# Block-local attention and two MoE layers on one core: scores moved to tiles 0, 2, 4 of every block, heads on 64 rows, two buffers for queries with keys and for values, low halves of w_in on VectorE

## The reference

```
q_c = q[:, :, c_start:c_end]                      # 4 x 8 heads, 768 tokens, head size 64
k_full = concat([mem_k, k[l_start:r_end]])        # 64 keys a chunk; v_full likewise
scores = scale * q_c @ k_full.T; scores -= max(scores)
a = exp(scores); a = a / (sum(a) + 1e-9); x_c = a @ v_full
h = x @ w_in                                      # 3072 x 512 @ 512 x 2048
g = h * cos(h);  y = g @ w_out                    # 2048 x 512
h2 = max(max(y @ w1, y @ w2), y @ w3)             # 512 x 768 each
out = h2 @ w_out2                                 # 768 x 512
```

## Time and profile before

| | |
|---|---|
| median of 3 runs | 1000.99 us (997.13 to 1005.64) |
| profiled execution | 1001.07 us, span 999.3 us |
| granted TensorE clock, mean | 0.991 |
| busy: TensorE, VectorE, ScalarE, GpSimd | 96%, 68%, 52%, 21% |
| first tile of block 0 starts | 30.71 us |
| last evacuation of the first stage | 393.6 us |

### The profile page before, as it was taken

One profiled execution on the slowest core, in us unless ns is written; L12 is line 12 of the kernel. 1 busy time (PEld: TensorE's weight loads), 2 busy tenths in 40 slices (PEclk: granted clock), 3 DMA queues, 4 the chain that ended last, 5 costly groups with the idle time before them and its releaser, 6 DMA issues.

```text
span 999.3 us, 18401 instructions
## 1 busy us (share of the span) xinstructions
PE 955.4 (96%) x7564; PEld 927.5 (93%) x7564; DVE 675.2 (68%) x926; ACT 516.5 (52%) x689; POOL 213.3 (21%) x231
## 2 busy tenths in 40 slices
PE   5779999999999999999999999999999999999998
PEld 4678889898989899999999999999999999999998
DVE  4355666566665678998998989866646446677761
ACT  1576786767777789443343335443323224344441
POOL 3341111112111221200200000763000001684510
PEclk7999999999999999999999999999999999999999
DMA  9993656574754444343445433332020121334532
GB/s 206 218 241 101 173 149 191 146 201 128 203 151 146 142 134 168 126 156 109 159 144 183 146 114 122 127 137 74 32 95 32 65 95 53 117 116 139 179 116 85
DMA packets 65395, 135.41 MB, mean 136 GB/s; under 512 B 5920, under 2 KB 27424, under 8 KB 65312
## 3 DMA queue, kind: packets, MB, share of 16 engines
q1 hardware_dynamic: 54944, 98.58, 33.8%
q0 software_dynamic: 10368, 35.66, 10.9%
HBM read 87.03 MB, written 47.19 MB: 134 GB/s over the span
## 4 chain that ended last, share of the span: by engine, by line
PE 72%; ACT 10%; DVE 8%; DMA 5%; issue 3%; SPq 2%; POOL 1%; DVEq 0%; ACTq 0%
PE ps L606 23%; PE ps L608 22%; PE ps L607 22%; DMA early_qk<-qk_in 2%; PE ps L622 2%; ACT work L912 2%; DMA g_dram<-work 2%; DVE work L1189 2%; ACT work L914 1%; DVE units L1226 1%; PE ps L647 1%; ACT work L907 1%; ACT work L904 1%; PE ps L656 1%; DVE ssum L1156 1%
## 5 line engine op out<-in xcount | busy, mean ns | idle before, releaser
L606 PE MATMUL ps<-units 128*128 128x384 f32 (+1 forms) x1940 | 609.4, 314 | 6.7 <-ACT work L1087 3.0
L608 PE MATMUL ps<-units 128*128 128x384 f32 (+1 forms) x1940 | 602.3, 310 | 0.0
L607 PE MATMUL ps<-units 128*128 128x384 f32 (+1 forms) x1940 | 601.8, 310 | 0.0
L606 PEld LDWEIGHTS ps<-units 128*128 128x128 f32 x1940 | 368.5, 190 | 17.5 <-issue 5.6
L607 PEld LDWEIGHTS ps<-units 128*128 128x128 f32 x1940 | 368.7, 190 | 0.0
L608 PEld LDWEIGHTS ps<-units 128*128 128x128 f32 x1940 | 368.6, 190 | 0.0
L932 ACT CAST units<-work 128x1024 fp32r<-128x1024 f32 x96 | 85.7, 939 | 119.0 <-DVE work L1212 102.8
L1087 ACT COPY work<-ps 128x384 f32<-128x384 f32 (+1 forms) x144 | 63.5, 454 | 144.0 <-PE ps L608 143.8
L1184 DVE SCALAR_TENSOR_TENSOR work<-work 128x768 f32<-128x768 f32 x64 | 62.1, 970 | 73.4 <-ACT work L907 73.4
L1226 DVE TENSOR_TENSOR units<-work,units 128x1024 fp32r<-128x1024 f32 x96 | 102.6, 1110 | 10.9 <-ACT units L932 10.9
L494 POOL DMA_DIRECT2D g_dram<-work x64 | 46.7, 730 | 292.0 <-DVE work L1189 287.3
(11 more groups left out here) (96 smaller groups left out, 840.7 us busy)
## 6 DMA issues: line engine op xcount, KB each, us to landing
g_dram<-work POOLq DMA_DIRECT2D x64, 384.0 KB, 3.2
work<-g_dram SPq DMA_DIRECT2D x48, 512.0 KB, 3.8
work<-qk_in SPq DMA_DIRECT2D x36, 384.0 KB, 5.5
work<-v_in SPq DMA_DIRECT2D x40, 256.0 KB, 5.1
work<-w_in POOLq DMA_DIRECT2D x40, 256.0 KB, 3.6
h_dram<-work SPq DMA_DIRECT2D x24, 384.0 KB, 2.9
work<-h_dram SPq DMA_DIRECT2D x18, 512.0 KB, 3.9
work<-y_dram SPq DMA_DIRECT2D x8, 768.0 KB, 6.0
```

The source lines that it names most:

```text
L606: pe.matmul(o, wh, mh, start=start, stop=False, skip_group_check=onto)
L607: pe.matmul(o, wh, ml, start=False, stop=False, skip_group_check=onto)
L608: return pe.matmul(o, wl, mh, start=False, stop=stop, skip_group_check=onto)
```

## The change

- A score and a value matmul serve one head on its own 64 rows, 32 moving matmuls a token tile instead of 16, each with 64 moving columns instead of 128. The two heads write two banks (4 and 5; scores in their first, weighted values in their second halves). No zeros are needed, the rows of queries and keys are packed (384 numbers a pair of heads), and a token tile's load is one DMA.
- Every block computes the scores of the next block's token tiles at its tiles 0, 2 and 4, the exponentials ahead of the evacuation at tile 5, the rest of the attention at tiles 7 to 13.
- Token tiles from 9 on use two buffers for queries with keys and two for values. The order of the loads is new.
- The transposed probabilities have one bank (6) after the start, the transposed output bank 7.
- `low_wi` runs on VectorE, in the order `LOW_WI`; `high_wi` runs in the order `HIGH_WI`, w_in tile g at tile f of block 0. GpSimd stores only.
- Some steps of the weights of the next stage move by a few tiles.

```diff
+HIGH_WI = (0, 0, 0, 0, 0, 0, 0, 0, 1, 1, 2, 3, 3, 4, 4, 4)
+LOW_WI = (0, 0, 0, 0, 0, 0, 1, 1, 2, 3, 3, 4, 5, 6, 6, 8)
...
+        def by_head(n, half):
+            if n == 1:
+                banks, at = ps[:, 0:2, :], 0
+            elif n == 2:
+                banks, at = ps[:, 2:4, :], 0
+            else:
+                banks, at = ps[:, 4:6, :], 256 * half if n else 0
+            return banks[:, :, at:at + 256].rearrange("p r (a k) -> p a r k", a=PAIRS)
...
-                        mm = pe.matmul(scores(n)[chunk, a, :, :], q[:, a, KC + CH * c:KC + CH * c + CH],
-                                       two_parts(q, a, c, KC + SUB), start=True, stop=True)
+                        for r in range(2):
+                            mm = pe.matmul(scores(n)[chunk, a, r, :], queries_in(n, a, r, c), keys_in(n, a, r, c),
+                                           start=True, stop=True)
...
-                        mm = pe.matmul(weighted(n)[chunk, a, :, :], prob_t(n)[:, a, chunk],
-                                       values_in(n, a, c), start=True, stop=True)
+                        for r in range(2):
+                            mm = pe.matmul(weighted(n)[chunk, a, r, :], prob_t(n)[head_rows(r), a, chunk],
+                                           values_in(n, a, r, c), start=True, stop=True)
...
             def load_qk(n):
...
-                for r, columns in enumerate((slice(0, KC + SUB), slice(KC, 2 * KC + SUB))):
-                    rows = slice(P // 2 * r, P // 2 * (r + 1))
-                    sp.dma_start(qk_at(n)[rows, :, columns], qk_in[n, rows, :].rearrange("p (a x) -> p a x", a=PAIRS))\
-                      .then_inc(qk_sem(n)[0], 16)
+                sp.dma_start(qk_at(n), qk_in[n, :, :].rearrange("p (a x) -> p a x", a=PAIRS)).then_inc(qk_sem(n)[0], 16)
...
             load_qk(0)
             load_qk(1)
             load_v(0)
-            load_wi(0)
             load_qk(2)
             load_v(1)
             load_v(2)
-            for f in range(1, 6):
+            for f in range(4):
                 load_wi(f)
             for n in range(NSUB, 2 * NSUB):
                 load_qk(n)
-                load_wi(2 * n)
-                load_wi(2 * n + 1)
...
+                load_wi(2 * n - 2)
+                load_wi(2 * n - 1)
+            load_wi(10)
+            load_wi(11)
+            load_v(NSUB)
+            load_wi(12)
+            load_v(NSUB + 1)
+            load_wi(13)
+            load_v(NSUB + 2)
+            load_wi(14)
+            load_wi(15)
...
+            def attend(t, f):
+                n = NSUB * (t + 1)
+                if f in (0, 2, 4):
+                    scores_of(n + f // 2, n)
                 elif f == 7:
                     turn_probs(n)
                 elif f == 9:
-                    values(n)
+                    values(n, n + 3)
                     turn_probs(n + 1)
                 elif f == 10:
                     turn_out(n)
                     turn_probs(n + 2)
                 elif f == 11:
-                    values(n + 1)
-                    scores_of(n + NSUB)
+                    values(n + 1, n + 3)
                 elif f == 12:
                     turn_out(n + 1)
-                    scores_of(n + NSUB + 1)
+                    values(n + 2, n + 3)
                 elif f == 13:
-                    values(n + 2)
-                elif f == 14:
                     turn_out(n + 2)
-                    scores_of(n + NSUB + 2)
...
             for t in range(NBLK):
                 n = NSUB * (t + 1)
...
+                    if not last and f == 5:
                         exps(0, NSUB, n + NSUB)
                     if f % 2:
                         i = FPAIRS * t + f // 2
                         evacuate(i)
...
+                        if not last:
+                            if f == 7:
+                                copy_probs(n)
+                            elif f == 9:
+                                copy_probs(n + 1)
+                            elif f == 13:
+                                x_high(n + 2)
                         if i:
                             cosine(i - 1)
-                    if first:
+                    if t == 0:
+                        for g in range(4, NF):
+                            if HIGH_WI[g] == f:
+                                high_wi(g)
+                    if not last:
                         if f == 10:
                             x_high(n)
                             copy_probs(n + 2)
                         elif f == 12:
                             x_high(n + 1)
...
-                    if 1 <= t < 6 and f == 10:
+                    if 1 <= t < 6 and f == 8:
                         high_w1(t - 1)
```

More of the change, by code:

```diff
@@ L555, in _ @@
             pool.wait_ge(const_ready, 1)
[L556 to L565, removed]
+            for i in range(TILES):
                 store_g(i)
                 t, p = divmod(i, FPAIRS)
-                if 1 <= t < 5 and p == 6:
+                if t < 5 and p == (6 if t else 4):
                     load_w1(t)
@@ L978, in _ @@
             copy_probs(0)
-            high_wi(0)
             exps(2, 3, 3)
             copy_probs(1)
+            copy_probs(2)
+            high_wi(0)
+            high_wi(1)
             x_high(0)
-            copy_probs(2)
+            high_wi(2)
+            high_wi(3)
             x_high(1)
             x_high(2)
-            for f in range(1, 5):
-                high_wi(f)
             for t in range(NBLK):
                 n = NSUB * (t + 1)
-                first, last = t == 0, t == NBLK - 1
+                last = t == NBLK - 1
                 for f in range(NF):
-                    if first and f + 5 < NF:
-                        high_wi(f + 5)
-                    if first and f == 5:
+                    if not last and f == 5:
                         exps(0, NSUB, n + NSUB)
@@ L1268, in _ @@
             sums(0, 1, 1)
+            sums(1, 2, 2)
             shift(2)
-            sums(1, 2, 2)
             normalise(0)
@@ L1273, in _ @@
             normalise(1)
+            low_wi(0)
             x_low(0)
             normalise(2)
+            low_wi(1)
             x_low(1)
             x_low(2)
+            low_wi(2)
+            low_wi(3)
             for t in range(NBLK):
                 n = NSUB * (t + 1)
-                first, last = t == 0, t == NBLK - 1
+                last = t == NBLK - 1
                 for f in range(NF):
-                    if first:
-                        if f == 0:
-                            shift(n)
-                        elif f == 2:
-                            shift(n + 1)
-                        elif f == 4:
-                            shift(n + 2)
-                        elif f == 8:
-                            sums(0, NSUB, NSUB + 1)
+                    if not last:
+                        if f in (0, 2, 4):
+                            shift(n + f // 2)
+                        elif f == 5:
+                            sums(0, NSUB, NSUB + t + 1)
                         elif f == 9:
@@ L1294, in _ @@
                             normalise(n + 1)
-                            shift(n + NSUB)
-                        elif f == 13:
-                            normalise(n + 2)
-                    elif not last:
-                        if f == 2:
-                            sums(0, NSUB, NSUB + t + 1)
-                        elif f == 3:
-                            normalise(n)
-                        elif f == 7:
-                            normalise(n + 1)
-                        elif f == 11:
-                            normalise(n + 2)
                     if f % 2:
@@ L1309, in _ @@
                         turn(i)
+                        if f == 13 and not last:
+                            x_low(n + 2)
                         if i:
                             gated(i - 1)
-                    if first:
+                    if not last:
                         if f == 10:
```

233 lines of the change are left out of this document (76 added, 157 removed).

## The result

| | before | after |
|---|---|---|
| median | 999.76 us (997.13 to 1005.64, 4 runs) | 975.38 us (974.13 to 976.64, 4 runs) |
| ratio to before | | 0.9752, interval 0.9716 to 0.9788 |
| profiled execution | 1001.07 us, span 999.3 | 974.13 us, span 972.3 |

What follows compares the result with a forecast made beforehand. TensorE, busy 96%, was taken to set the pace after about 70 us, with full transfers before. Terms of -11, -5.4 and +1.4 gave -15 against 1001.07 us: 986 us, range 978 to 1018.

Steps and rivals of the forecast that it cites:

- Part 3: Start and block 0: 1.4 us more, bounds 4 us less to 6 more.
- the landing of w_in: Start: last part of w_in lands at 58 us again, bounds 55 and 61.
- What hung on that term: Block 0: ScalarE's conversions of w_in, last at 58.6 us, then exponentials and evacuation (62.9), so tile 8 starts at 63.
- the idle time before it: Block 0: TensorE idle for 14 us before tile 8.
- Rival D: Start: w_in's last pair lands at 62 to 65 us and holds ScalarE longer; time 1004 to 1008, chance 0.13.
- Part 1: Scores and values on 64 rows: slot of a group 0.7 us, down from 1.01, 36 times, 11 us less.
- rivals B and C: Score and value groups: B, row halves take turns, 997 us, chance 0.22; C, records set the pace, 1011 to 1029, 0.18.
- Part 2: New order in blocks 1 to 6: 2 us less, 1 less in each of 2 to 5, 0.6 more; 5.4 less in sum.
- the wait for VectorE: Blocks 1 to 6: the output's transposes no longer wait, as the normalisation comes at 14.4 us, before they want it at 14.5.
- the copy's wait: Blocks of the new order: the third probabilities' transposes wait for ScalarE's copy, a new wait of 1.5 us.
- the values' wait: Blocks of the new order: copy of the probabilities done at 10.95 us, wanted by the values at 10.9.

Runs made afterwards that it cites:

- halves: Kernel after, with each load of queries and keys or of values as two DMAs, on the lower and the upper 64 rows: 990.16 us, ratio 0.9912.
- evenodd: Kernel after, with each such load as two DMAs of 64 rows, one on the even and one on the odd rows: 976.54 us, ratio 0.9764.
- small: Kernel after, with queries and keys loaded over all 128 rows in pieces of 1.5 KB: 975.11 us, ratio 0.9755.
- before_two_queues: Kernel before, with DMAs of the upper 64 rows of token tiles 0 to 5 issued by ScalarE's queue: 1003.72 us, ratio 1.003.
- before_even_odd: Kernel before, with head 0 on even and head 1 on odd rows, zeros written ahead of the first loads: 996.78 us, ratio 0.9963.
- w1_at_10: Kernel after, with the high part of w_out back from tile 8 to tile 10 of blocks 1 to 5: 970.43 us, ratio 0.969.
- before_even_odd_low: before_even_odd with the low halves of w_in on VectorE, at tile g-4 of block 0: 996.26 us, ratio 0.9962.

## Why the prediction was wrong

*The step that failed* is the size of one term in Part 3, the landing of w_in: "rows of 6 KB instead of 1.5 save some ... 15% of 4.7 MB, 2.5 us. So 58 again; bounds 55 and 61". It landed at 37. The 209 and 244 GB/s of the earlier trace rows were taken as the chip's rate, for which only the size of rows was a possible difference. But both stretches were full of DMAs that wrote only the lower or only the upper 64 rows, and these go at half the rate. The change lists "a token tile's load is one DMA"; that one line was costed as saved issues. `halves` and `evenodd` isolate it at some 15 us of the 24, `small` shows that the size of rows is worth nothing. The Trainium skill has the rule, in "SBUF — State Buffer", section "Door 1: The DMA port swizzle": which of SBUF's 16 ports a transfer reaches depends on the numbers of its rows, and rows 0 to 63 reach only 8 of them, as do 64 to 127. This case agrees with it: 227 GB/s for the halves, 407 for even and odd rows, which by that rule reach all 16. The section "Can I just issue two DMAs to hit both halves?" of the same page of the Trainium skill says that two DMAs, one on either half, measured only 6% over one. `before_two_queues` gained a fifth of the rate, and, as said there, tests that only in part. The trace of before answers the question without it, in slices of 0.25 us from 20 to 30 us:

```profile
DMA  9799999999999999999999999999999999999999
GB/s 246 180 279 221 221 205 238 221 164 148 131 139 164 262 369 402 385 434 361 360 369 377 369 375 324 182 176 143 137 143 150 188 162 201 209 221 240 240 219 219
```

The engines are busy throughout, but from 23.5 to 26 us they move 360 to 434 GB/s. Five tiles of w_in, which write all 128 rows, were issued together at 9.17 to 11.65 and landed 15 to 18.5 us later, and 431 of the 526 packets of this stretch have 2 KB or more, as w_in's rows have; the 1.5 KB of queries and keys are few. The mean of 244 over ten microseconds hid a stretch at nearly the rate of the kernel after.

*What hung on that term* was right, as `halves` shows to a microsecond from the last conversion to tile 8; the idle time before it was 7.3 us and not 14. Rival D looked for a later landing; none looked for an earlier one, and the lower bound of part 3, 4 us less, was too near: it was 18.

*The gain needs both halves of the change.* Faster loads alone are worth 3 to 4 us (`before_even_odd`; perhaps 6, an estimate, had its first load not been issued 2.3 us later), the new order, matmuls and buffers alone 9.5 (`halves`), both 24.4. In the old order the start and block 0 are held by other things just behind the loads: the chain of the first attention (first tile at 29.98 against 26.5, of which 2.3 may be the later first load) and VectorE with GpSimd.

*Part 1* held: 64 records in 0.79 us, within 0.6 to 0.9, so rivals B and C fell; 36 x 0.225 = 8 us in place of 11, since only the first 32 records go at 7 ns and the rest at 12 to 13. Of the two rules on small matmuls that the prediction takes from the Trainium skill, that of 25 ns between starts is refuted for tiles of different rows and columns (7 ns), and that of 4 ns is nearer, but no more than nearer.

*Part 2* held in its mechanism and was too large in its size: the wait for VectorE went, the copy's wait came at 1.1 us (1.5 forecast), but the values' wait of up to 0.7 us (0.05 forecast) was not counted. Block 1 gained 1.6 us of order (2 forecast: 46.5 to 43.6, less six slots of 0.225), blocks 2 to 5 0.5 each by their windows (1 forecast). `w1_at_10` shows that the new wait had the cause that was named. Block 6 grew from 42.0 to 42.6 us instead of losing 1.3: its three added groups of scores cost 2.4, the shorter groups of values give back 0.7, and TensorE's waits in it fell only from 1.9 us (1.6 and 0.3) to 0.7. Why the later stages took 1.2 more stays open.

*What stays open:* what two queues reach when both halves of every load are issued together; what faster loads alone are worth without the late first load; why the pace of the records falls after 32; and the last 1.7 us that `before_even_odd_low` wins in the first stage and its span doesn't show.

## What to carry to other kernels

Where the DMA share is at 1, divide: if the GB/s are far below what other stretches or kernels reach at the same share, look at which rows each DMA writes before you look at its sizes; here one DMA over all rows, or over every second, went at nearly twice the rate of one over 64 neighbours. Look at the rate in slices shorter than the loads, too: a mean can hide the fast stretch. A forecast made along a chain of waits is only as good as the rate at its head, so give that rate a bound on either side and a rival each way. And a load that comes earlier pays only if nothing else stands just behind it: look for the next wait before you count the gain.

## What had not been expected of the hardware

- 64 neighbouring rows: 227 GB/s; 64 even or odd rows: 407; 128 rows in pieces of 1.5 KB: 386 (10 to 20 us, DMA share 1.02 to 1.05 in each).
- Matmuls of 64 rows x 32 columns, alternating between row halves and column groups, start 7 ns apart for the first 32 records, then 12 to 13 ns on the average.
- While GpSimd runs subtractions of 512 columns, an addition of VectorE's to 24 numbers a row takes 1.89 us in place of 0.18, and a turn of 0.96 takes up to 3.36.
